# Partial products chained in PSUM by a ScalarE copy, in place of additions on VectorE

## The reference, cut to what matters

```python
h = x @ w_in                      # 512 -> 2048
y = np.maximum(0.01 * h, h) @ w_out   # 2048 -> 512
a = y @ w1                        # 512 -> 1024
b = y @ w2
out = ((a * b) @ w3) @ w_out2     # 1024 -> 1024 -> 512
```

## Time and profile before

| | us |
|---|---|
| median of 3 runs | 512.49 |
| lowest, highest | 512.42, 512.62 |
| the profiled execution | 512.28 |
| its span | 510.4 |
| TensorE busy | 505.6 |
| VectorE busy | 355.2 |
| ScalarE busy | 200.8 |
| GpSimd busy | 93.2 |

### The profile page before, as it was taken

How to read it: one execution, slowest core, us unless ns; L and a number is a source line. 1 busy time by engine, 2 the same in 40 slices (tenths; PEclk the granted TensorE clock), 3 DMA queues, 4 the chain that set the end, 5 groups by cost and what they waited for, 6 DMA issues and landing times.

```text
span 510.4 us, 9091 instructions
## 1 busy us (share of the span) xinstructions
PE 505.6 (99%) x3568; PEld 417.5 (82%) x3568; DVE 355.2 (70%) x537; ACT 200.8 (39%) x356; POOL 93.2 (18%) x101
## 2 busy tenths in 40 slices
PE   8999999999999999999999999999999999999997
PEld 6888888888888888888888888888888888888886
DVE  4667356767786876877665777697777755878962
ACT  5364243343556433333311546443333214473420
POOL 2223132111122311333300020323333300000000
PEclk9999999999999999999999999999999999999999
DMA  8999582534121111111000031212221116240012
GB/s 278 345 393 334 170 297 85 159 125 127 42 84 42 42 41 42 42 42 41 5 38 0 22 83 34 77 52 88 57 89 63 41 43 205 82 166 0 13 50 103
DMA packets 27065, 51.57 MB, mean 101 GB/s; under 512 B 4232, under 2 KB 4496, under 8 KB 27024
## 3 DMA queue, kind: packets, MB, share of 16 engines
q1 hardware_dynamic: 24560, 43.53, 25.7%
q10 hardware_dynamic: 2432, 7.47, 4.4%
q0 software_dynamic: 32, 0.00, 0.0%
HBM read 45.74 MB, written 5.25 MB: 100 GB/s over the span
## 4 chain that ended last, share of the span: by engine, by line
PE 99%; DVE 0%; issue 0%; DVEq 0%
PE acc L1438 12%; PE acc L1440 11%; PE acc L1439 11%; PE hid L1639 10%; PE hid L1638 10%; PE hid L1637 10%; PE hid L1438 7%; PE hid L1439 7%; PE hid L1440 7%; PE hid L1467 1%; PE hid L1482 1%; PE hid L1495 1%; PE acc L1764 1%; PE acc L1763 1%; PE acc L1765 1%; PE hid L1506 1%
## 5 line engine op out<-in xcount | busy, mean ns | idle before, releaser
L1438 PE MATMUL acc<-g_hi,wb 128*128 128x512 f32 x224 | 87.6, 391 | 0.0
L1439 PE MATMUL acc<-g_lo,wb 128*128 128x512 f32 x224 | 87.2, 389 | 0.0
L1440 PE MATMUL acc<-g_hi,wb 128*128 128x512 f32 x224 | 87.2, 389 | 0.0
L710 POOL TENSOR_TENSOR w_in_lo_place<-stage 128x256 f32<-128x256 f32 x16 | 12.6, 788 | 211.6 <-PE hid L1639 121.7
L1438 PE MATMUL hid<-xy_hi,wa_hi 128*128 128x512 f32 x128 | 50.3, 393 | 0.0
L1440 PE MATMUL hid<-xy_hi,wa_lo 128*128 128x512 f32 x128 | 49.8, 389 | 0.0
L1439 PE MATMUL hid<-xy_lo,wa_hi 128*128 128x512 f32 x128 | 49.8, 389 | 0.0
L1637 PE MATMUL hid<-wa_hi 128*128 128x512 f32 x128 | 49.8, 389 | 0.0
L1638 PE MATMUL hid<-wa_lo,wa_hi 128*128 128x512 f32 x128 | 49.8, 389 | 0.0
L1639 PE MATMUL hid<-wa_hi,wa_lo 128*128 128x512 f32 x128 | 49.8, 389 | 0.0
L1438 PEld LDWEIGHTS acc<-g_hi,wb 128*128 128x128 f32 x224 | 42.0, 188 | 8.9
(11 more groups left out here) (222 smaller groups left out, 931.1 us busy)
## 6 DMA issues: line engine op xcount, KB each, us to landing
stage<-weights SPq DMA_DIRECT2D x109, 256.0 KB, 3.0
w_out_place<-attn ACTq DMA_DIRECT2D x12, 512.0 KB, 4.9
x_hi_place<-attn SPq DMA_DIRECT2D x4, 512.0 KB, 8.9
w_out_place<-attn SPq DMA_DIRECT2D x4, 512.0 KB, 7.8
w_dram<-x_lo_place SPq DMA_DIRECT2D x8, 256.0 KB, 4.4
stage<-w_dram SPq DMA_DIRECT2D x8, 256.0 KB, 2.7
x_lo_place<-attn SPq DMA_DIRECT2D x2, 512.0 KB, 6.5
x_hi_place<-attn ACTq DMA_DIRECT2D x2, 512.0 KB, 6.4
```

Source lines behind the costliest of these rows:

```text
L710: nc.gpsimd.tensor_tensor(s_1, a21, a22, ALU.add).then_inc(s_made, 1)
L1438: nc.tensor.matmul(out, w_hi, a_hi, start=first, stop=False)
L1439: nc.tensor.matmul(out, w_hi, a_lo, start=False, stop=False)
L1440: return nc.tensor.matmul(out, w_lo, a_hi, start=False, stop=final)
```

## The change

ScalarE now copies the first product from X into the Y bank (PSUM), and TensorE adds S2 T2, S3 T3 and A22 T4 onto it, so that Y holds the sum at each of the three moments. `join_u2`, one of the two additions of `join_u3`, and `join_s1` go. ScalarE gains three copies a step: S1 T1 from Z to SBUF (`copy_p5`), U2 out of Y (`copy_u2`), and the third result scaled (first block) or the X quarter (second block). U3 is Y plus the copy of S1 T1, on VectorE. TensorE does S1 T1 second and S2 T2 third; T1 is split ahead of T2. One matmul with `start=True` is added into the Y bank in step 0. ScalarE's weight casts are placed between its copies.

```diff
--- before.py
+++ after.py
...
-T_SPLIT = [T2, T2, T1, T1, T3, T3, T4, T4]
+T_SPLIT = [T1, T1, T2, T2, T3, T3, T4, T4]
...
                     nc.scalar.copy(wa_hi[:, slot], w_in_lo_place[:, slot, :].rearrange("p (k m) -> p k m", k=KD_TILES)).then_inc(s_hi_done, 1)
-            def copy_s1(e, place):
+            def copy_s1(e):
                 act.wait_ge(x_ready, 2 * e + 1)
-                nc.scalar.copy(place, bank(X_BANKS[e % 3])).then_inc(s1_copied, 1)
+                nc.scalar.copy(bank(Y_BANK), bank(X_BANKS[e % 3])).then_inc(s1_copied, 1)
+            def copy_p5(e, p5):
+                act.wait_ge(z_ready, 2 * e + 1)
+                act.wait_ge(u3_made, e)
+                nc.scalar.copy(p5, bank(Z_BANKS[e % 3])).then_inc(p5_copied, 1)
+            def copy_u2(e, u2):
+                act.wait_ge(y_ready, 3 * e + 1)
+                act.wait_ge(z_used, e)
+                if e < F2:
+                    act.wait_ge(g2_ready, 2 * e)
+                else:
+                    act.wait_ge(g1_ready, e - F2)
+                nc.scalar.copy(u2, bank(Y_BANK)).then_inc(u2_copied, 1)
             def round_gated(n, ready, f, source):
                 act.wait_ge(ready, f)
...
                         j += 1
             for e in range(F2):
+                if e > 0:
+                    act.wait_ge(g_ready, CREDIT_G + F1 + 2 * e)
+                copy_s1(e)
                 if e == 0:
                     act.wait_ge(t_made, SUMS_OF_X)
-                else:
-                    act.wait_ge(g_ready, CREDIT_G + F1 + 2 * e)
-                copy_s1(e, joins(2)[0])
+                copy_p5(e, joins(2)[0])
                 if e + 1 < F2:
-                    for _ in range(2):
-                        weight_hi(w)
-                        w += 1
-                    s_hi(e + 1)
+                    weight_hi(w)
+                copy_u2(e, joins(2)[1])
+                if e + 1 < F2:
+                    weight_hi(w + 1)
+                    w += 2
                 act.wait_ge(x_ready, 2 * e + 2)
                 act.wait_ge(g_split, F1 + 2 * e + 1)
                 nc.scalar.mul(g[:, 0, :], bank(X_BANKS[e % 3]), LEAK).then_inc(scaled, 1)
+                if e + 1 < F2:
+                    s_hi(e + 1)
                 round_hidden(F1 + 2 * e)
+                act.wait_ge(y_ready, 3 * e + 3)
+                act.wait_ge(g_split, F1 + 2 * e + 2)
+                nc.scalar.mul(g[:, 1, :], bank(Y_BANK), LEAK).then_inc(scaled, 1)
                 if e == 0:
                     copy_y(0)
                 elif e <= 2:
...
             for f in range(F2):
                 if f == 0:
+                    act.wait_ge(g_ready, CREDIT_G + 2 * F1)
                     act.wait_ge(t_made, SUMS_OF_X + SUMS_OF_Y)
                 else:
                     act.wait_ge(g0_ready, f)
-                copy_s1(F2 + f, joins(1)[0])
-                for _ in step_order(f):
+                copy_s1(F2 + f)
+                copy_p5(F2 + f, joins(1)[0])
+                weight_hi(w)
+                copy_u2(F2 + f, joins(1)[1])
+                w += 1
+                act.wait_ge(x_ready, 2 * (F2 + f) + 2)
+                act.wait_ge(g_split, N1 + f + 1)
+                nc.scalar.copy(g[:, f % 2, :], bank(X_BANKS[(F2 + f) % 3])).then_inc(quarter_copied, 1)
+                for _ in step_order(f)[1:]:
                     weight_hi(w)
                     w += 1
                 if f + 1 < F2:
...
-            def join_u2(e, s1, u2):
-                dve.wait_ge(s1_copied, e + 1)
-                dve.wait_ge(y_ready, 3 * e + 1)
-                nc.vector.tensor_tensor(u2, bank(Y_BANK), s1, ALU.add).then_inc(y_used, 1)
-
-            def join_u3(e, s1, u3):
+            def join_u3(e, p5, u3):
+                dve.wait_ge(p5_copied, e + 1)
                 dve.wait_ge(y_ready, 3 * e + 2)
-                nc.vector.tensor_tensor(u3, bank(Y_BANK), s1, ALU.add).then_inc(y_used, 1)
-                dve.wait_ge(y_used, 3 * e + 2)
-                dve.wait_ge(z_ready, 2 * e + 1)
-                nc.vector.tensor_tensor(u3, bank(Z_BANKS[e % 3]), u3, ALU.add).then_inc(z_used, 1)
-
-            def join_s1(e, s1):
-                dve.wait_ge(y_ready, 3 * e + 3)
-                nc.vector.tensor_tensor(s1, bank(Y_BANK), s1, ALU.add).then_inc(y_used, 1)
-                dve.wait_ge(y_used, 3 * e + 3)
+                nc.vector.tensor_tensor(u3, bank(Y_BANK), p5, ALU.add).then_inc(u3_made, 1)
             def join_z(e, u2):
+                dve.wait_ge(u2_copied, e + 1)
                 dve.wait_ge(z_ready, 2 * e + 2)
                 nc.vector.tensor_tensor(u2, bank(Z_BANKS[e % 3]), u2, ALU.add).then_inc(z_used, 1)
-                dve.wait_ge(z_used, 2 * e + 2)
+                dve.wait_ge(z_used, e + 1)
             def leaky_of(out, exact, done):
                 nc.vector.scalar_tensor_tensor(out, exact, LEAK, exact, ALU.mult, ALU.max).then_inc(done, 1)
...
                     dve.wait_ge(acc_done, CREDIT_G + F1 + g2_slot(f) + 1)
                 leaky_of(g2(f), exact, g2_ready)
-            s1, u2, u3 = joins(2)
+            p5, u2, u3 = joins(2)
             for e in range(F2):
                 if e > 0:
                     dve.wait_ge(g2_ready, 2 * e)
-                join_u2(e, s1, u2)
                 if e + 1 < F2:
                     for _ in range(2):
                         weight_lo(w)
                         w += 1
-                dve.wait_ge(scaled, F1 + e + 1)
+                dve.wait_ge(scaled, F1 + 2 * e + 1)
                 nc.vector.tensor_tensor(g[:, 0, :], g[:, 0, :], bank(X_BANKS[e % 3]), ALU.max).then_inc(g_ready, 1)
-                join_u3(e, s1, u3)
-                dve.wait_ge(z_used, 2 * e + 1)
+                join_u3(e, p5, u3)
+                dve.wait_ge(u3_made, e + 1)
                 leaky_later(2 * e + 1, u3)
                 if e + 1 < F2:
                     s_lo(e + 1)
-                join_s1(e, s1)
-
-                dve.wait_ge(g_split, F1 + 2 * e + 2)
-                leaky_of(g[:, 1, :], s1, g_ready)
                 split_hidden(F1 + 2 * e)
+                dve.wait_ge(scaled, F1 + 2 * e + 2)
+                nc.vector.tensor_tensor(g[:, 1, :], g[:, 1, :], bank(Y_BANK), ALU.max).then_inc(g_ready, 1)
                 join_z(e, u2)
                 leaky_later(2 * e, u2)
                 split_hidden(F1 + 2 * e + 1)
...
                     t_lo(j, len(T_SPLIT))
                     j += 1
-            s1, u2, u3 = joins(1)
+            p5, u2, u3 = joins(1)
             for f in range(F2):
                 e = F2 + f
                 if f > 0:
                     dve.wait_ge(g1_ready, f)
-                join_u2(e, s1, u2)
                 for _ in step_order(f):
                     weight_lo(w)
                     w += 1
-                join_u3(e, s1, u3)
+                join_u3(e, p5, u3)
                 if f + 1 < F2:
                     s_lo(e + 1)
-                join_s1(e, s1)
-                dve.wait_ge(x_ready, 2 * e + 2)
-                nc.vector.tensor_tensor(g[:, f % 2, :], s1, bank(X_BANKS[e % 3]), ALU.mult).then_inc(g0_ready, 1)
+                dve.wait_ge(y_ready, 3 * e + 3)
+                dve.wait_ge(quarter_copied, f + 1)
+                nc.vector.tensor_tensor(g[:, f % 2, :], g[:, f % 2, :], bank(Y_BANK), ALU.mult).then_inc(g0_ready, 1)
                 if f == 0:
                     last_y_lo()
                 join_z(e, u2)
+                dve.wait_ge(u3_made, e + 1)
                 nc.vector.tensor_tensor(g1(f), u2, u3, ALU.mult).then_inc(g1_ready, 1)
                 split_hidden(N1 + f)
...
                 name = ("pair", 2 * e + 1) if e < F2 else ("w12", 2 * (e - F2) + 1)
                 pe.wait_ge(split_done, CREDIT_SPLIT + PLACE[name] + 1)
                 if e > 1:
-                    pe.wait_ge(z_used, 2 * (e - 1))
+                    pe.wait_ge(z_used, e - 1)
+                if e == 0:
+                    nc.tensor.matmul(y_bank, wa_hi[:, set_slot(0, 0), 0, :], xy_hi[:, 0, tokens(t)], start=True, stop=True)
                 small_product(x_bank, e, A11, B11, t, True).then_inc(x_ready, 1)
                 pe.wait_ge(s_split, 2 * e + 1)
                 if e % F2 == 0:
                     pe.wait_ge(t_split, 2 if e < F2 else len(T_SPLIT) + 2)
-                if e > 0:
-                    pe.wait_ge(y_used, 3 * e)
-                small_product(y_bank, e, S2, T2, t, True).then_inc(y_ready, 1)
                 pe.wait_ge(*x_used)
+                small_product(z_bank, e, S1, T1, t, True).then_inc(z_ready, 1)
                 if e % F2 == 0:
                     pe.wait_ge(t_split, 4 if e < F2 else len(T_SPLIT) + 4)
-                small_product(z_bank, e, S1, T1, t, True).then_inc(z_ready, 1)
                 pe.wait_ge(s1_copied, e + 1)
+                small_product(y_bank, e, S2, T2, t, False).then_inc(y_ready, 1)
                 small_product(x_bank, e, A12, B21, t, False).then_inc(x_ready, 1)
                 pe.wait_ge(s_split, 2 * e + 2)
```

(19 more changed lines are left out.)

## The result

| | before | changed |
|---|---|---|
| median, us | 512.42 | 517.20 |
| lowest, highest | 512.00, 512.62 | 516.03, 517.32 |
| span of the profiled execution | 510.4 | 515.5 |
| VectorE busy | 355.2 | 326.3 |
| ScalarE busy | 200.8 | 227.2 |

Six runs each. The ratio is 1.0091, 95% interval 1.0081 to 1.0102: slower by 4.8 us. VectorE lost 29 us of work and nothing was gained by it.

The account below looks back on a forecast made before the run. TensorE, busy 505.6 of 510.4 us, was taken to bound the kernel. Added matmul and second-block gaps, 0.23 + 6 x 0.83 + 0.23 = 5.44 us, gave 517.9 us against the median 512.49, range 516.5 to 520.0.

Parts of the forecast that it names:

- The bound: Both blocks: TensorE is busy throughout, so VectorE's freed 2.1 us a step gives back 0.
- The two holding waits: TensorE's waits for the S1 copy (0.59 us, 0.24 to spare) and the U2 copy (ends 4.93 against 5.22) cost nothing.
- The thin place behind the first step: ScalarE's queue at the first step's end: next S1 copy ends 14.65, needed 14.74; counted 0, upper end 0.1 us.
- The wait that does not hold: Second block, sixth product waits for join_u3, queued behind lower parts: gap 0.83 us in six steps, 0.23 in step 6.
- the end of the chain: Second block: join_u3 ends at 8.72, TensorE can load at 8.77 and wants to at 7.94, gap 0.83 us.
- The sum: Added matmul plus second-block gaps: 0.23 + 6 x 0.83 + 0.23 = 5.44 us.
- The matmul: One added start flag matmul for the Y bank in the first step: +0.23 us.
- the seven restarts: TensorE resuming after the gaps in second-block steps 0 to 6: six gaps of 0.83 us, one of 0.23.
- Covers hold: Rival: join_u3 starts by 7.19 instead of 8.03, so only the added matmul costs, 512.7 us; chance 0.05.
- A slow write into PSUM: Rival: ScalarE's S1 copy exceeds 0.83 us, each 0.1 past it costing 1.6 us; 524.3 at 1.23; chance 0.05.
- The clock: Rival: gaps let TensorE's clock fall to 1.2 GHz, adding 9.5 us, 527.4 us; chance 0.02.

Follow-up runs that it names:

- the mended versions: Changed kernel, second block, one move each: VectorE's join_u3 ahead of the second lower part, 512.42 us (1.0004); ScalarE's casts ahead of the X quarter copy, 512.48 us (0.9998).
- the run with two copies: Changed kernel with ScalarE making the S1 copy twice in a row in both blocks, the second waiting for the first: 522.41 us (1.0194 of before).
- before with late casts: Kernel before, with only ScalarE's second and third weight casts of a second-block step made to wait for the fourth product: 513.81 us (1.0035).
- the version with join_u3 first: Changed kernel with VectorE's join_u3 moved ahead of the second lower part of the weights in the second block: 512.42 us (1.0004 of before).

## Why the prediction was right, point by point

**The bound.** That only TensorE's starts count, that the freed time of VectorE gives nothing back and that both blocks have no gap to win: right. VectorE is down by 29 us and the mended versions stand at 1.0004 and 0.9998 of before. From the second product of the first step to that of the last, TensorE's starts lie 248.88 us apart in before and in both mended versions.

**The two holding waits.** The S1 copy writes PSUM in 0.57 us (15 of 16; 0.59 was taken), the U2 copy is in time, and the first block has no wait. On this the Trainium skill ("ScalarE: Activation LUTs", Step-by-step: what each stage is for) was right in direction: 0.570 us into PSUM against 0.587 into SBUF from the same banks. The thin place behind the first step held. ScalarE in the changed kernel there (line 987 scales the sum, 851 copies banks, 839 rounds):

```profile
173.68 0.60 ACT L987 ACTIVATE g<-hid 128x512 f32<-128x512 f32 x1 [3.29 <-PE hid L1659]
174.18 2.05 ACT L851 COPY x_lo_place<-acc 128x512 f32<-128x512 f32 x4
176.07 0.67 ACT L839 CAST g_hi<-g 128x512 fp32r<-128x512 f32 x1
176.59 0.64 ACT L884 COPY hid<-hid 128x512 f32<-128x512 f32 x1
```

```profile
177.34 0.39 PE L1659 MATMUL hid<-wa_hi,wa_lo 128*128 128x512 f32 x1
177.56 0.39 PE L1657 MATMUL hid<-wa_hi 128*128 128x512 f32 x1
```

The S1 copy starts at 176.59, which is 0.39 us behind the start of the next product; in other steps it is 0.25. So it is 0.13 late, where I had laid out 0.20, and it takes 0.64. TensorE's third product starts at 177.56, at the usual spacing behind the matmul of 177.34: the place costs nothing, the value that I counted. The S1 copies mislead here. From the first of the block to the third it is 27.26 us instead of 27.20, but only because the first one starts 0.20 behind the next product and not 0.25; by TensorE's starts it is 27.20 in both kernels.

**The wait that does not hold.** Place, cause and chain were right, each start within 0.06 us: the X quarter at 5.64 for 5.70, the casts at 6.12 and 6.64 for 6.18 and 6.70, join_u3 at 7.99 for 8.03. The term that was mis-sized is the end of the chain. I let TensorE load its weights at 8.77 and then wait out its usual 0.22 before the first matmul, a start at 8.99. Load and matmul both start at 8.73, and only the next matmul is late by 0.11. So the gap is 0.70 and not 0.83, in five steps; by TensorE's starts 0.78 in the first, where TensorE follows VectorE's end by 0.14 and not 0.06; 0.10 and not 0.23 in the seventh; none in the last. The list of waits therefore names six, the longest 0.5, where I had written some seven and 0.8; the seventh is too short for it.

**The sum.** In the trace of the changed kernel TensorE's starts of the second product in the first and the last step of the second block are 90.06 us apart (327.16 to 417.22), in before 85.68 (326.39 to 412.07): 4.38 for the predicted 5.21. The matmul is 0.23 as predicted, the thin place 0. That is 4.6 us, and 4.8 were measured. The forecast of 5.4 was above it by the seven restarts, each taken too long. The spans of the two profiled executions differ by 5.1; the 0.5 that the sum lacks there lies ahead of the blocks, as the last point tells.

**The rivals.** Covers hold: no, but it is what the mended versions give. A slow write into PSUM: no, by the copies' rows and by the mended versions; its threshold, put at 0.83, comes out at 0.87 by the run with two copies. The clock: 1.00 in the window with the gaps, so pauses that cost 0.7 us in every 12.9 us do nothing to it here. The rule of the Trainium skill ("TensorE: Matmul & The Clock Gate", A second HAM failure mode: psum-queue depth-cycling) on an oscillating clock does not apply to this spacing by these runs.

**What stays open.** The profiled executions differ ahead of the blocks. The first S1 copy is at 162.95 to 163.52 in before, in the two mended kernels and in before with late casts, at 163.36 to 164.90 in the changed kernel and its variants, and at 165.79 with nine start matmuls, 1.8 of which are theirs. Their programs are the same up to there but for the order of T's halves. Between before and the changed kernel TensorE has lost 0.28 us by 21 us, where it waits for the first weights (the third row of the waits above, 0.6 us), and the rest at 96 us, in the row that names "issue" (0.5 for 0.3). No run was made on either, and the cause is open. It is why single times carry some 0.5 us that the steps do not.

## What to carry to other kernels

When one engine bounds the kernel, an edit that takes work from another engine can only be judged by the waits of the first: list each wait that it gains or keeps, and for each the chain of instructions queued ahead of the one that releases it, with start distances and not durations. Work that has no hurry (here the weights of the next step) must not stand between the bounding engine and what it waits for while its own inputs are late: put it behind, as VectorE's order does in one mended version, or make its inputs early, as ScalarE's does in the other. Moving one instruction past two others was worth 4.8 us. The list of waits leaves out gaps shorter than the stretch by which a matmul's row reaches over the next start (0.39 - 0.227 = 0.16 us); the distance between equal starts of successive steps shows them to 0.01 us. Take the starts of the bounding engine itself: those of another engine, here the S1 copies, carry their own lateness.

## What the runs showed of the hardware that I had not expected

- Behind a wait TensorE's weight load and first matmul start together, 0.06 us after VectorE's end (372.69 + 0.68 to 373.43; 0.14 in the first step of the second block, 334.48 to 334.62), and the next matmul comes 0.34 us on instead of 0.227. From VectorE's end to where the first matmul would have had to start for a step of that length it is 0.19 to 0.22 us, not the 0.27 that I took for word and load.
- The hand-over from TensorE isn't one number per engine. ScalarE starts the S1 copy 0.26 us behind its product and the X quarter 0.20 behind its own (370.14 to 370.34 in the changed kernel), and the S1 copy of the very first step follows by 0.20 as well; VectorE's read for U3 came 0.20 behind in before and 0.27 behind in the version with join_u3 first (368.68 to 368.95). The cause is open.
